# Constant waits with self-emptied semaphores in the second pass of a recurrent attention, and the output-weight split spread over the first dense block

## What is computed

```python
for t in range(S):
    y[:, :, t] = np.einsum('bhd,bhde->bhe', rt, state)
    Sa = np.einsum('bhde,bhe->bhd', state, at)
    state_decay = state * wt[:, :, None, :] - np.einsum('bhd,bhe->bhde', Sa, bt)
    state = state_decay + np.einsum('bhd,bhe->bhde', vt, kt)
```

## Time and profile before

| what | before |
| --- | --- |
| device time, median of 3 runs | 1130.01 us (1127.5 to 1132.26) |
| the profiled execution | 1133.65 us, of which the span of instructions is 1131.5 us |
| PE / PEld / DVE / ACT / POOL busy | 86% / 77% / 55% / 27% / 29% of the span |
| second pass, 24 steps of PE | 164.1 to about 413 us |
| dense stage | 754.8 to 1131.5 us |
| mean granted clock of PE | 0.988 |

### The profile page before, as it was taken

One profiled execution on the slowest core, in us unless ns is written; L12 is line 12 of the kernel. 1 busy time (PEld: TensorE's weight loads), 2 busy tenths in 40 slices (PEclk: granted clock), 3 DMA queues, 4 the chain that ended last, 5 costly groups with the idle time before them and its releaser, 6 DMA issues. The chain is left out here.

```text
span 1131.5 us, 44178 instructions
## 1 busy us (share of the span) xinstructions
PE 976.8 (86%) x19565; PEld 870.8 (77%) x19566; DVE 625.4 (55%) x999; ACT 301.0 (27%) x698; POOL 326.5 (29%) x411
## 2 busy tenths in 40 slices
PE   3402348999999987999999999998999999999997
PEld 3302338888988975888888888867899999999996
DVE  8999976889787753111111111125656666666654
ACT  5412434555455530110110110121222222222211
POOL 1682998898930003114611100023101000000000
PEclk9999999999899998999999999999999999999999
DMA  7823875888688627997884444512010001010100
GB/s 223 230 75 105 218 224 156 256 253 245 197 250 251 187 68 239 306 287 248 239 261 159 149 155 157 158 38 68 24 24 24 24 1 24 1 24 1 24 1 23
DMA packets 114617, 158.32 MB, mean 140 GB/s; under 512 B 59092, under 2 KB 87652, under 8 KB 114180
## 3 DMA queue, kind: packets, MB, share of 16 engines
q1 hardware_dynamic: 104276, 127.28, 37.2%
q0 software_dynamic: 5824, 25.28, 7.5%
q10 hardware_dynamic: 4464, 5.08, 1.4%
HBM read 131.98 MB, written 19.23 MB: 134 GB/s over the span
## 5 line engine op out<-in xcount | busy, mean ns | idle before, releaser
L909 DVE TENSOR_SCALAR ht<-h_bank 128x512 f32<-128x512 f32 x62 | 42.9, 692 | 266.6 <-PE h_bank L874 253.3
L874 PEld LDWEIGHTS h_bank<-xt,w 128*128 128x128 f32 x1488 | 172.8, 194 | 8.2 <-issue 3.4
L874 PE MATMUL h_bank<-xt,w 128*128 128x128 f32 x1488 | 173.1, 277 | 3.2 <-issue 3.2
L642 PE MATMUL bank<-alpha,second 40*64 40x64 f32 x1568 | 45.1, 271 | 111.0 <-DVE alpha L392 111.0
L887 PE MATMUL y_bank<-w_all,ht 128*128 x496 | 138.7, 433 | 0.0
L1134 ACT CAST g_hi<-g 128x512 fp32r<-128x512 f32 x96 | 59.5, 620 | 279.6 <-DVE g L1094 273.7
L642 PEld LDWEIGHTS bank<-alpha,second 40*64 40x64 f32 x1568 | 39.2, 180 | 113.5 <-issue 113.5
L1027 PE MATMUL y_bank<-w_out_hi,g_hi 128*128 128x320 f32 x384 | 119.3, 311 | 2.2 <-DVE g_lo L1077 1.2
L127 POOL TENSOR_TENSOR solved<-solved,share 128x31 f32<-128x31 f32 (+15 forms) x155 | 117.6, 759 | 12.1
L124 POOL TENSOR_TENSOR share<-solved,blk 128x31 f32<-128x31 f32 (+15 forms) x155 | 115.3, 744 | 12.2
L1027 PE MATMUL y_bank<-w_out_hi,g_lo 128*128 128x320 f32 x384 | 118.7, 309 | 0.0
(11 more groups left out here) (169 smaller groups left out, 1653.1 us busy)
## 6 DMA issues: line engine op xcount, KB each, us to landing
w<-w_in SPq DMA_DIRECT2D x31, 1024.0 KB
t_in<-wab_in SPq DMA_DIRECT2D x24, 776.0 KB, 6.6
t_in<-wak_in SPq DMA_DIRECT2D x24, 776.0 KB, 5.4
w_all<-w_in POOLq DMA_DIRECT2D x8, 1280.0 KB, 9.0
rr<-rr_in SPq DMA_DIRECT2D x24, 384.0 KB, 3.2
w<-w_in SPq DMA_DIRECT2D x31, 256.0 KB
vt<-vt_in SPq DMA_DIRECT2D x24, 256.0 KB, 3.3
vtm<-vtm_in SPq DMA_DIRECT2D x24, 240.0 KB
```

Of the source, the lines that this page charges most:

```text
L642: last = pe.matmul(out[HALF * to:HALF * to + rows_out, row, n * i:n * i + n], lhs, rhs, start=opens and i == 0, stop=closes and i == HP - 1)
L874: last = pe.matmul(h_bank[s][f // FH][:, f % FH * ET:(f % FH + 1) * ET], w1[s][:, k, f * PARTS:(f + 1) * PARTS], xt[s][:, k, :], start=k = ...
L909: dve.tensor_scalar(ht[s][:, FH * n:FH * n + FH, :].rearrange("q f t -> q (f t)"), h_bank[s][n][:, :], 0.0, None, ALU.max).then_inc(s_relu, 1)
```

## The change

Five edits:

1. In the second pass PE waits for constants. `heads` and `picks` get a list `takes` of (semaphore, count): PE waits for each count, and the first matmuls of the group subtract it again when they finish. 21 of the 22 `arrive` go; the one on `s_alpha` stays. In the built program two constant waits for one group stand in a single semaphore instruction: a step has 15 of them on PE where it had 22, and no register arithmetic for the wait on s_vtm and on the later st. 21 matmuls of a step carry a subtraction that they did not carry before.
2. `out_of["y"]` and `s_ready` now rise and fall, so SP can't compare them with a growing number. `cross_wq` waits for `did["s"]` and `load_inverses` for `did["u"]`, each with the old number.
3. The first memset of swt and the last `gates_of` use other semaphores.
4. In the dense stage DVE makes v_lo parts 0 and 1 at the start, part 2 after g_lo of j = 0 and part 3 after g_lo of j = 3; `outputs` waits for a part when it first needs it.
5. `idle(8)` becomes `idle(5)` there.

```diff
             def load_inverses(k):
                 if k >= 2:
-                    sp.wait_ge(s_ready, k - 1)
+                    sp.wait_ge(did["u"], k - 1)
...
             def cross_wq(k):
                 sp.wait_ge(s_wc, STEPS + k + 1)
                 if k >= 2:
-                    sp.wait_ge(out_of["y"], k)
+                    sp.wait_ge(did["s"], k)
...
-            def heads(product, out, n, opens=True, closes=True, done=None):
+            def heads(product, out, n, opens=True, closes=True, done=None, takes=()):
+                for sem, count in takes:
+                    pe.wait_ge(sem, count)
+                left = list(takes)
...
+                        if left:
+                            sem, count = left.pop(0)
+                            last.then_inc(sem, -count)
...
-                arrive(s_ax, 32 * i)
-                arrive(out_of["st"], i)
-                heads(alpha_s, BA, DIM, closes=False)
-                arrive(out_of["g2"], i)
-                arrive(s_vtm, 16 * i)
-                heads(g2_v, BA, DIM, opens=False, done="w")
-                arrive(out_of["y"], i)
-                heads(turned_state, BB, DIM, done="s")
...
-                arrive(out_of["w"], i)
-                arrive(s_ready, i)
-                heads(u_product, BC, DIM, done="u")
...
+                heads(alpha_s, BA, DIM, closes=False, takes=[(s_ax, 32)])
+                heads(g2_v, BA, DIM, opens=False, done="w", takes=[(s_vtm, 16), (out_of["g2"], 1)])
+                heads(turned_state, BB, DIM, done="s", takes=[(out_of["y"], 1)])
...
+                heads(u_product, BC, DIM, done="u", takes=[(s_ready, 1), (out_of["w"], 1)])
...
-                if j == 0:
-                    pe.wait_ge(s_vlo, 4)
+                if b == 0 and f % STEP == 0:
+                    pe.wait_ge(s_vlo, f // STEP + 1)
...
-            idle(8)
+            idle(5)
...
-            for n in range(4):
+            def low_v(n):
...
+            low_v(0)
+            low_v(1)
...
                 low_g(j)
+                if j in (0, 3):
+                    low_v(2 + j // 3)
```

More of the change, by code:

```diff
@@ L353, in _ @@
             dve.memset(restart[:, :, WIDE - 1:WIDE], 1.0).then_inc(s_set, 1)
-            dve.memset(swt[:, :, :], 0.0).then_inc(out_of["st"], 1)
+            dve.memset(swt[:, :, :], 0.0).then_inc(s_set, 1)
             dve.memset(yt[:, :, :], 0.0)
@@ L404, in gates_of @@
                 gates = BD[:, :, 0:QP * PICK].rearrange("q h (p e) -> q e h p", e=PICK)[:, DIM:PICK]
-                dve.tensor_reduce(logit[:, k, :], gates, mybir.AxisListType.XY, ALU.add).then_inc(out_of["pick"], 1)
+                return dve.tensor_reduce(logit[:, k, :], gates, mybir.AxisListType.XY, ALU.add)
             def masked(dst, src):
@@ L432, in _ @@
                     if k >= 2:
-                        gates_of(k - 2)
+                        gates_of(k - 2).then_inc(out_of["pick"], 1)
                     else:
@@ L463, in _ @@
                     masked(g2, BC).then_inc(out_of["g2"], 1)
-            gates_of(STEPS - 2)
+            gates_of(STEPS - 2).then_inc(out_of["pick"], 1)
             y_out(STEPS - 1)
-            gates_of(STEPS - 1)
-            dve.wait_ge(out_of["pick"], STEPS + 2)
             link = chain(dve, s_v)
+            link(gates_of(STEPS - 1))
             def each(t, n):
@@ L698, in sat_product, with picks @@
                 return (q ^ m, q, DIM) + inverted(i, q, m)[::-1]
-            def picks():
+            def picks(takes=()):
+                for sem, count in takes:
+                    pe.wait_ge(sem, count)
+                left = list(takes)
                 for p in range(QP):
@@ L724, in _ @@
             pe.wait_ge(keep.s_gw, 32)
+            pe.wait_ge(s_set, 3)
             with pe.Fori(1, STEPS + 1) as i:
-                arrive(s_ax, 32 * i)
-                arrive(out_of["st"], i)
-                heads(alpha_s, BA, DIM, closes=False)
-                arrive(out_of["g2"], i)
-                arrive(s_vtm, 16 * i)
-                heads(g2_v, BA, DIM, opens=False, done="w")
-                arrive(out_of["y"], i)
-                heads(turned_state, BB, DIM, done="s")
-                arrive(out_of["pick"], i)
@@ L735, in _ @@
-                heads(turned(second), BD, DIM, done="ktm")
-                arrive(out_of["w"], i)
-                arrive(s_ready, i)
-                heads(u_product, BC, DIM, done="u")
-                arrive(out_of["s"], i)
-                arrive(out_of["ktm"], i)
-                heads(from_s(lambda i, q, m: eye(m)), BD, DIM, closes=False)
-                heads(from_k(lambda i, q, m: at_m(vtm, i, q, m, rows(m))), BD, DIM, opens=False, closes=False)
-                arrive(out_of["u"], i)
@@ L744, in _ @@
[L744 to L750, removed]
-                heads(sat_product, BA, C, done="sat")
-                arrive(out_of["m1"], i)
-                heads(from_s(lambda i, q, m: at_m(rr, i, q, m, live(m))), BB, C, closes=False)
@@ new lines, in _ @@
+                heads(turned(second), BD, DIM, done="ktm", takes=[(out_of["pick"], 1)])
+                heads(u_product, BC, DIM, done="u", takes=[(s_ready, 1), (out_of["w"], 1)])
+                heads(from_s(lambda i, q, m: eye(m)), BD, DIM, closes=False, takes=[(out_of["s"], 1), (out_of["ktm"], 1)])
+                heads(from_k(lambda i, q, m: at_m(vtm, i, q, m, rows(m))), BD, DIM, opens=False, closes=False)
+                heads(low_part, BA, DIM, done="z", takes=[(s_off, 1), (out_of["u"], 1)])
@@ new lines, in _ @@
+                heads(m1_product, BB, C, done="m1", takes=[(s_vt, 16), (s_rr, 16)])
+                heads(sa_product, BC, DIM, done="sa", takes=[(out_of["z"], 1)])
+                heads(sat_product, BA, C, done="sat")
+                heads(from_s(lambda i, q, m: at_m(rr, i, q, m, live(m))), BB, C, closes=False, takes=[(out_of["m1"], 1)])
+                heads(from_b(lambda i, q, m: sa_tm[rows(m), slot(q ^ m, i), :]), BD, DIM, opens=False, done="st", takes=[(s_btm, 1), (out_of["sa"], 1)])
+                heads(m2_product, BA, C, done="m2", takes=[(out_of["sat"], 1)])
@@ L761, in _ @@
                 heads(from_k(lambda i, q, m: m1[rows(m), slot(q, i), :]), BB, C, opens=False, closes=False)
[L762 to L767, removed]
+                picks(takes=[(out_of["st"], 1)])
+                heads(from_b(lambda i, q, m: m2[rows(m), slot(q, i), :]), BB, C, opens=False, done="y", takes=[(out_of["m2"], 1)])
+            pe.wait_ge(out_of["y"], 1)
+            pe.wait_ge(out_of["pick"], 1)
             picks()
```

## The result

| | median us | lowest to highest | runs |
|---|---|---|---|
| before, beside the changed kernel | 1131.13 | 1127.50 to 1134.45 | 4 |
| changed kernel | 1146.58 | 1143.03 to 1147.89 | 4 |

The change makes the kernel slower: 1.0132 times the time before, with a 95% interval of 1.0092 to 1.0172. The profiled execution of the changed kernel took 1146.23 us and has a span of 1144.0.

What follows compares the result with a forecast made beforehand. PE and SP almost balanced (9.53 against 9.92 a step), SP's issue chain to ax deciding. 1133.65 + 12.6 - 0.8 - 2.4 = 1143.1, less 3.6 gives 1139.5 for the median; own range 1133 to 1145, full range 1126 to 1148.

Steps and rivals of the forecast that it cites:

- SP's later start (edit 2): Second pass: wqx waits for s, leaving at 1.55 not 0.71; everything behind moves 0.84, 18 steps take 12.6 us more.
- The clock: Second pass, 18 steps: one step stays at the low clock, 13.1 and not 10.3, adding 2.8 us.
- the first rival: Second pass: PE's idling makes the clock fall more often; three more falls, +7.5 us, so 1147; chance 0.18.
- PE's own path (edit 1): Second pass: fewer wait instructions take 0.35 us off PE's own path in a step, 9.53 to 9.18.
- the saving at u: Second-pass step: one wait instruction fewer, 0.16 us, ends u earlier, and this is passed on along the path to z.
- The subtractions: Second pass: subtractions on PE's matmuls cost zero; the skill's 26 ns each, some 1.9 us over 18 steps, left out.
- The transfers and not the issues set the landing: Second pass: ax lands when the queues have emptied, so starting 0.84 later costs nothing: no change, 1127.6; chance 0.20.
- PE's own path ends last: Second pass: later start absorbed, ax there by 9.0 after step start, 0.35 kept per step: 1119.2; chance 0.12.
- The dense stage: Dense stage: hidden(0) starts 3.1 us earlier, 0.7 given back at outputs(1); net -2.4 us, bounds -3.1 and 0.

Runs made afterwards that it cites:

- e6: The changed kernel plus five matmuls nobody reads behind y in every second-pass step: median 1143.79 us, ratio 1.0122 to the kernel before.
- e2: The kernel before with only SP's waits changed to did s and did u: median 1153.17 us, ratio 1.0191.
- e3: The changed kernel with SP's old waits, and PE's old waits for y and s_ready: median 1124.13 us, ratio 0.9953 to the kernel before.
- e4: The changed kernel with ax, vtm and vt issued ahead of row stores and block transfers on SP: median 1122.62 us, ratio 0.9915 to the kernel before.
- e1: The kernel before with only the dense-stage changes (v_lo parts moved, five idle matmuls): median 1129.49 us, ratio 0.9992.
- e5: The kernel before with the dense-stage changes and ax, vtm and vt issued early on SP: median 1123.13 us, ratio 0.9920.
- e7: e3 with ax, vtm and vt issued early on SP, as in e4 and e5: median 1119.12 us, ratio 0.9898 to the kernel before.
- e8: e5 plus 22 unread semaphore updates a step on second-pass matmuls: 1123.96 us in one run.
- e9: e5 plus unread updates on all matmuls of each group but the last, 255 a step: 1190.78 us in one run.

## Why the prediction was right in its sign and short in its size

It said slower, 1139.5 with its own range to 1145 and a full range of 1126 to 1148; the time is 1146.58. So the direction and the mechanism hold, and the loss came out at 15.4 us in the medians where 9.5 was forecast. The miss of 7.1 has two halves. From one profiled execution to the other, 1143.1 was forecast and 1146.23 measured, 3.1 short, with 4.2 in the 18 steps (194.3 against 198.49) and some of it regained elsewhere. The other half is the 3.6 that the sum took off at its end, because the profiled execution of before was that much above its median. The changed kernel's lies 0.35 below its own, so this subtraction had no ground.

**SP's later start (edit 2): right.** wqx was put at 1.55 after the step's start and left at 1.59. For a step like the one at 315.27 the sum gave 10.58; it took 10.56. For one with both blk and tt_mid it gave 11.1; the two of them at a full clock took 11.00 and 11.16, and in the two others the clock fell (12.27 and 11.44). With a full clock the 18 steps were put at 191.5, and e6, where the clock is full, has 193.0, with some steps held up by its own added work. PE's waits for ax were to go to 25 or more: 26.3. e2 shows that this edit alone does it, e3 that nothing is lost without it, and e4 that it is the place of ax in the queue that makes it expensive.

**The clock: the mis-sized term.** The sum kept one step at a low clock, at a cost of 2.8 us. In the changed kernel there were five stretches at the lower level (1.2 GHz), 37.5 us together, each in another step. e6 measures at least 5.5 us for them, so the term was at least 2.7 too small, the larger part of the 4.2; the other 1.5 is the part at a full clock, 193.0 in e6 (with e6's own added work) against 191.5. This is the first rival's mechanism. Its price was 7.5 us for three more falls; there were four more, and at least 2.7 us. That its 1147 lies so near to the time measured is partly luck, since it too has the 3.6 taken off. What PE did before shows in its row at a step's start, here for three of the five:

```profile
257.99 0.30 PE L644 MATMUL bank<-swt,alpha 40*64 40x40 f32 x1 [1.59 <-DMA ax<-alpha]
```

```profile
282.17 0.30 PE L644 MATMUL bank<-swt,alpha 40*64 40x40 f32 x1 [2.22 <-DMA ax<-alpha]
```

```profile
368.59 0.22 PE L644 MATMUL bank<-swt,alpha 40*64 40x40 f32 x1 [2.96 <-DMA ax<-alpha]
```

The other two had pauses of 1.81 and 1.83, and the 13 steps that kept their clock had 1.39 or less. The prediction asked for a pause of 2 or more, by the single fall that the trace of before has the earlier trace rows, and so counted too few steps. It isn't a rule either: in e2 pauses of 1.61, 2.23 and 2.62 went by without a fall, and one of 1.31 had one. What holds over the runs is the tendency: e2 with 28.4 us of waits for ax has five stretches, the changed kernel with 26.3 five, e3 (6.8 in the steps from the third on) and the kernel before (8.2) one each, e1 (5.4) none, and e4, e5, e7 and e8, without such waits there, none. Against it stands e9: no wait for ax from the third step on, a pause of 0.25, and yet the clock was at 0.87 in the step from 295.25. Why it fell there stayed open. The forecast and this rival weren't alternatives; the second rides on the first. I gave it 0.18 as if a coin decided, and should have put a part of it into the sum.

**PE's own path (edit 1): 0.22, not 0.35.** Unheld steps went from 9.53 to 9.31 (e3, e4, e7); the forecast was 9.18, "under 9.3". The failed step is that the saving at u is passed on to z. u's loads do begin earlier, 0.84 after those of s (316.20 to 317.04) instead of 1.00, just the 0.16 that I took. But the next product (eye,st) needs the copy of ktm, and ACT does w_tm, st and ktm one after the other:

```profile
316.50 0.43 ACT L605 COPY w_tm<-bank 128x320 f32<-128x320 f32 x1 [2.17 <-PE bank L644]
316.82 0.43 ACT L607 COPY st<-bank 128x320 f32<-128x320 f32 x1
317.31 0.42 ACT L609 COPY ktm<-bank 128x320 f32<-128x320 f32 x1
```

ktm is copied by 317.73, and the loads that wait for it begin at 317.85, 1.65 after those of s, as they did before (308.78 after 307.13). So the saving at u is taken back there. The wait after ax landed did fall as predicted, from 0.26 to 0.10.

**The subtractions: right, for their number.** 22 updates cost nothing (e8), and steps of 9.31 come with all of them in place. The Trainium skill ("TensorE: Matmul & The Clock Gate", section "The cost: per-tile semaphore tail") has updates on matmuls in line, some 26 ns each. e9 shows such a line, at 42.5 ns each, when nearly every matmul carries one. It does not show as long as they are few, so the +1.9 us that the rule would have given was rightly left out.

**The transfers and not the issues set the landing: fell.** In the changed kernel the DMA share of the 18 steps went down, 0.79 to 0.72, and landing times stayed at 2.3 to 4.4 with a median of 2.6. So ax landed later by as much as it was issued later: the emptier queues gave nothing back. In e4, with ax issued 2.6 earlier and ahead of other transfers, it landed 7.4 to 9.3 after the start of a step instead of 9.9 to 12.2. Late landings came as before, 3.6 in the step from 270.76 and 4.4 in the one from 356.44 (12.12 us).

**PE's own path ends last: not in this kernel, and its price agrees by luck.** It was put at 1119.2 with the condition that ax comes 1.5 us earlier. e7 creates the condition by the order on SP, and takes 1119.12. But the rival took 0.35 a step for 24 steps from the time before, and left out that the 18 steps stood 10.2 us above 18 times 9.53. Measured were 0.22 a step and 12.8 us in the 18 steps (181.70 to 168.87), beside a kernel before whose median was 1133.34 and not 1130.0.

**The dense stage: right within 0.2 us.** -2.4 was forecast and -2.2 measured. Two errors cancelled. I had shared the time of eight idle matmuls out evenly, but they begin at the lower level of the clock and end at the higher one, as the stretch from 769.90 and the loads of their halves show:

```profile
769.90:773.30 3.40, 3.40 (x5) 1.34 (x5) 2.39 (x2) 3.40 (x4) 2.62 (x2) 0.50 0.17 48
...
771.28 0.34 PEld L993 LDWEIGHTS h_bank<-w_out_sb,ones 128*128 128x128 f32 x1 [0.52 <-issue]
772.13 0.34 PEld L993 LDWEIGHTS h_bank<-w_out_sb,ones 128*128 128x128 f32 x1 [0.52 <-issue]
...
774.42 0.19 PEld L993 LDWEIGHTS h_bank<-w_out_sb,ones 128*128 128x128 f32 x1 [0.24 <-issue]
774.85 0.19 PEld L993 LDWEIGHTS h_bank<-w_out_sb,ones 128*128 128x128 f32 x1 [0.24 <-issue]
```

The three that went were fast ones: six halves of 0.43 are 2.6 us, and `hidden(0)` came 2.6 earlier and not 3.1. Only 0.4 was given back instead of 0.7.

## What to carry to other kernels

A wait on a queue costs what stands behind it: look for the last transfer that the next step needs, and count the issues up to it, here twelve or thirteen in a row of half a microsecond each. Before you judge a wait expensive, try to move that transfer forward; here that was worth more than all waits that the change made cheaper. And where a change makes the matmul engine idle at the same place in each round, count the clock as part of the cost from the start. When you count matmuls in a trace, look in the kernel for how many records each of them has.

## What the runs showed of the hardware

**The clock rises late in the second pass, and the stretches don't show it.** In all traces the loads of the second pass begin at a slow rate, in its first step, and the moment at which the rate rises differs from run to run. e4's second step is the clearest:

```profile
184.12:198.55 14.43, 14.43 (x587) 14.28 (x579) 8.88 (x14) 5.52 (x13) 13.18 (x17) 1.00 0.46 133
```

```profile
191.18 0.99 PEld L645 LDWEIGHTS bank<-w_tm,inv 64*64 64x64 f32 x32
```

PE is busy for the whole of the step, and 32 loads take 0.99 us where they take 0.59 elsewhere. The row has 1.00 as its clock, but the trace has no record of the clock there, and the view counts time without a record as full. The trace's first clock record is a stretch at full clock from 199.6 on in e4, from 185.0 in the kernel before, 182.8 in the changed one, 192.5 in e2 and e9, 180.0 in e6, 176.1 in e7 and 175.6 in e3, and in each trace the loads quicken at that moment. And where the record does have the lower level, as in the changed kernel's step from 257.96 (0.60), the same 32 loads are as slow:

```profile
261.01 1.02 PEld L644 LDWEIGHTS bank<-w_tm,inv 64*64 64x64 f32 x32
```

So PE ran at the lower level up to that first record. In e4 it did so for 34.3 us of the pass, in e7 for 14.4, in the kernel before for 20.9. In e4 no pause of PE longer than 0.3 us is left between 182.0 and the rise at 199.6. The first two steps take 33.25 us in e4, 27.8 in e5 and 27.2 in e7, and this is why e4's faster steps give no shorter profiled execution than e5's. Whether SP's new waits make the rise late or chance does, these runs, with one trace of each, don't tell: e2 and e4 have these waits, but so have the changed kernel and e6, where it came early, and e9, without them, had it at 192.5. The Trainium skill ("TensorE: Matmul & The Clock Gate", section "What's actually happening") lets the engine start at 1.2 GHz and says that the moment of the rise varies from run to run. The traces agree with both, but the moment varies by far more here than the half microsecond to either side that the page gives: from 13.5 us into the pass (e3) to 34.3 (e4).

**Updates on matmuls have a pace, not a price:** 42.5 ns from one to the next once nearly every matmul has one (e9), nothing seen if 22 are spread over 288 matmuls (e8).

**Landings of ax vary, 1.9 to 4.4 us for the same transfer,** with a median of 2.4 to 2.7 in all kernels but one. In e9, whose steps of 12.38 leave the DMA engines at a share of 0.65, all landings from the third step on took 1.9 to 2.1. What makes the long ones elsewhere stayed open. With ax early there is room for them.
